# First four attention jobs with unpadded loads and a reordered opening, in a fused linear-attention and two-MLP kernel

## The reference

```python
f = 1.0 / (1.0 + np.exp(-f_logit))
for t in range(S):
    state = f[:, :, t, :, None] * state + np.einsum('bhd,bhe->bhde', k[:, :, t], v[:, :, t])
    y[:, :, t] = np.einsum('bhd,bhde->bhe', q[:, :, t], state)
x = tokens(y)    # (3072, 384)
r = np.maximum(x @ w_in, 0.0);  x = (r * r) @ w_out            # first MLP
h = x @ w_in2;  out = (h * np.tanh(softplus(h))) @ w_out2      # second MLP
```

## Time and profile before

| | |
|---|---|
| median of three runs | 887.02 us |
| the profiled execution's own time | 886.69 us |
| its span, first to last instruction | 885.0 us |
| around the span (886.69 - 885.0) | 1.69 us |
| TensorE matmul busy | 874.3 us, 99% |
| VectorE, ScalarE busy | 597.2 and 594.8 us, 67% each |
| granted TensorE clock | 1.00 |

### The profile page before, as it was taken

The page is one execution under the profiler, slowest core; times in us unless marked ns, Lnnn a source line. Parts: engine busy times, 40 slices in busy tenths (PEclk is TensorE's granted clock), DMA queues, the critical chain, the costliest instruction groups (busy, mean ns, idle before and its releaser), DMA issues.

```text
span 885.0 us, 16260 instructions
## 1 busy us (share of the span) xinstructions
PE 874.3 (99%) x6282; PEld 725.3 (82%) x6282; DVE 597.2 (67%) x1054; ACT 594.8 (67%) x1026; POOL 62.0 (7%) x71
## 2 busy tenths in 40 slices
PE   8899999999999999999999999999999999999998
PEld 7788888888888888888788888888888888888886
DVE  6879545445544444342244799999898898898886
ACT  6776655564546555544566787888887887877874
POOL 0222111111111111110000000000000000000000
PEclk9999999999999999999999999999999999999999
DMA  9644221122212111100233201001001001000100
GB/s 255 203 148 128 76 81 44 44 81 65 66 45 80 44 44 57 46 13 1 92 96 100 90 19 37 37 0 37 37 1 37 36 1 37 36 0 1 36 1 36
DMA packets 25090, 50.64 MB, mean 57 GB/s; under 512 B 2674, under 2 KB 3442, under 8 KB 25010
## 3 DMA queue, kind: packets, MB, share of 16 engines
q1 hardware_dynamic: 25010, 49.56, 18.0%
HBM read 40.11 MB, written 9.44 MB: 56 GB/s over the span
## 4 chain that ended last, share of the span: by engine, by line
PE 98%; DMA 1%; issue 0%; SPq 0%; ACT 0%; DVE 0%; ACTq 0%
PE ps L1069 45%; PE ps L1086 44%; PE ps L1043 2%; PE ps L1013 2%; PE ps L1039 2%; PE ps L991 1%; PE ps L1059 1%; DMA work<-fkq 1%; SPq L284 0%; PE ps L988 0%; PE ps L997 0%; SPq L297 0%; ACT work L497 0%; ACT work L538 0%; SPq L306 0%
## 5 line engine op out<-in xcount | busy, mean ns | idle before, releaser
L1069 PE MATMUL ps<-xs,w_hi 128*128 128x512 f32 x1152 | 359.3, 393 | 1.0 <-issue 1.0
L1069 PEld LDWEIGHTS ps<-xs,w_hi 128*128 128x128 f32 x1152 | 213.0, 188 | 45.0 <-issue 1.6
L1086 PE MATMUL ps<-g_hi,w_lo 128*128 128x512 f32 x576 | 224.1, 389 | 0.0
L1069 PE MATMUL ps<-xs,w_lo 128*128 128x512 f32 x576 | 224.1, 389 | 0.0
L1086 PE MATMUL ps<-g_hi,w_hi 128*128 128x512 f32 x576 | 224.1, 389 | 0.0
L1086 PE MATMUL ps<-g_lo,w_hi 128*128 128x512 f32 x576 | 224.1, 389 | 0.0
L829 DVE TENSOR_TENSOR g_lo<-gb,g_hi 128x512 fp32r<-128x512 f32 x96 | 68.1, 709 | 215.6 <-ACT gb L564 215.6
L559 ACT ACTIVATE rb<-ps 128x512 f32<-128x512 f32 x96 | 57.3, 597 | 161.0 <-PE ps L1069 161.0
L1069 PEld LDWEIGHTS ps<-xs,w_lo 128*128 128x128 f32 x576 | 108.1, 188 | 22.6
L1086 PEld LDWEIGHTS ps<-g_hi,w_hi 128*128 128x128 f32 x576 | 108.1, 188 | 22.5
L1086 PEld LDWEIGHTS ps<-g_hi,w_lo 128*128 128x128 f32 x576 | 108.1, 188 | 22.4
(11 more groups left out here) (82 smaller groups left out, 750.6 us busy)
## 6 DMA issues: line engine op xcount, KB each, us to landing
work<-fkq SPq DMA_DIRECT2D x68, 224.0 KB, 3.7
stage<-w SPq DMA_DIRECT2D x24, 384.0 KB, 3.1
work<-v_tok SPq DMA_DIRECT2D x22, 256.0 KB, 3.9
x_scratch<-yo SPq DMA_DIRECT2D x6, 768.0 KB, 3.8
xs<-x_scratch SPq DMA_DIRECT2D x6, 768.0 KB, 4.4
out<-work SPq DMA_DIRECT2D x17, 256.0 KB, 2.1
yo<-w SPq DMA_DIRECT2D x8, 384.0 KB, 4.6
work<-f_tok SPq DMA_DIRECT2D x4, 224.0 KB, 3.5
```

The costliest lines, as they stand in the source:

```text
L1069: ins = nc.tensor.matmul(bank, w[:, f, k * P:(k + 1) * P], xs[:, half, part, k, :], start=k == 0 and i == 0, stop=k == KT - 1 and i == 2)
L1086: ins = nc.tensor.matmul(ps[:, 5 + d, :], w[:, f, cols], g[:, slot, :], start=f == 0 and i == 0, stop=f == NF - 1 and i == 2)
```

## The change

- Decays of the first four jobs are loaded without padding (128 x 384), and `sums` makes two matmuls for a pair of heads in place of one: 64 columns for rows 0 to 63, 48 for rows 64 to 111, in different column parts of the array.
- Keys and queries of the first four jobs come from a new input `kq_first`, as two loads of 48 partitions each. VectorE first zeroes the gap of the key and query tiles (partitions 32 to 63, 1024 and 1536 elements each), and SP waits for that (`gap_zeroed`).
- Values of all jobs have 112 columns for a pair (48 of the even head, 16 shared zeros, 48 of the odd head) in place of 128.
- SP's order becomes f0 f1 k0 f2 q0 k1 f3 q1 v0 q2 k2 v1 k3 q3 w0 v2 v3; then it waits until v2 has landed before w1, and until v3 has landed before w2.
- VectorE zeroes `am` and `st` after `first_cap(1)` and not at the start, and `first_cap(2)` moves behind `first_queries(0)`.
- ScalarE copies keys(2) and keys(3) out right after their transposes, into `eb`; the wait for increments that this copy had moves to `inverse_decay`.
- TensorE runs `increments(1)` right behind `increments(0)`, ahead of `values(2)`.

```diff
...
+    DP = D + DV
...
-    VALUES = [(0, D), (DV - D, DV)]
+    VALUES = [(0, D), (DV, DP)]
...
-        vb, o = place(o, 2, H, DV)
+        vb, o = place(o, 2, NP, DP)
...
         def f_rows(j):
-            return (fb if j < 2 else eb)[:, j % 2, :, :].rearrange("p n t -> p (n t)")[:, 0:NP * R]
+            return (fb if j < 2 else eb)[:, j % 2, :, :].rearrange("p n t -> p (n t)")[:, 0:DM]
+        def loads(j, places):
+            before = range(j % places, j + 1, places)
+            return 16 * len(before) + 16 * len([i for i in before if i < B])
         def key_rows(j):
+            if j in (2, 3):
+                return eb[:, j % 2, :, :].rearrange("p n t -> p (n t)")[:, 0:NP * R].rearrange("p (n r) -> p n r", r=R)
...
         def v_rows(j):
-            return gb[:, j - 2, :].rearrange("p (h c) -> p h c", c=DV) if j in (2, 3) else vb[:, j % 2, :, :]
+            return gb[:, j - 2, 0:NP * DP].rearrange("p (n c) -> p n c", c=DP) if j in (2, 3) else vb[:, j % 2, :, :]
...
             def load_k(j):
                 if j < NJ:
...
-                    sp.dma_start(kb[0:R, j % 2, :, :].rearrange("p n t -> p (n t)"),
-                                 fkq[j][:, 1, :]).then_inc(k_in[j % 2], 16)
+                    if j < B:
+                        sp.wait_ge(s_["gap_zeroed"], 1)
+                        for e, (lo, hi) in enumerate(PAR):
+                            sp.dma_start(kb[lo:hi, j % 2, :, :].rearrange("p n t -> p (n t)"), kq_first[j, 0, e]).then_inc(k_in[j % 2], 16)
+                    else:
+                        sp.dma_start(kb[0:R, j % 2, :, :].rearrange("p n t -> p (n t)"),
+                                     fkq[j][:, 1, :]).then_inc(k_in[j % 2], 16)
             def load_q(j):
                 if j < NJ:
...
-                    sp.dma_start(qb[0:R, j % 3, :, :].rearrange("p n t -> p (n t)"),
-                                 fkq[j][:, 2, :]).then_inc(q_in[j % 3], 16)
+                    if j < B:
+                        sp.wait_ge(s_["gap_zeroed"], 2)
+                        for e, (lo, hi) in enumerate(PAR):
+                            sp.dma_start(qb[lo:hi, j % 3, :, :].rearrange("p n t -> p (n t)"), kq_first[j, 1, e]).then_inc(q_in[j % 3], 16)
+                    else:
+                        sp.dma_start(qb[0:R, j % 3, :, :].rearrange("p n t -> p (n t)"),
+                                     fkq[j][:, 2, :]).then_inc(q_in[j % 3], 16)
             def load_v(j):
                 if j < NJ:
...
-                    sp.dma_start(v_rows(j).rearrange("p h c -> p (h c)"), v_tok[j % B][t:t + C, :]).then_inc(v_in[j if j < B else j % 2], 16)
+                    sp.dma_start(v_rows(j).rearrange("p n c -> p (n c)"), v_tok[j % B][t:t + C, :]).then_inc(v_in[j if j < B else j % 2], 16)
...
             load_f_tok(0)
             load_f_tok(1)
+            load_k(0)
             load_f_tok(2)
-            load_k(0)
             load_q(0)
+            load_k(1)
             load_f_tok(3)
-            load_k(1)
             load_q(1)
+            load_v(0)
             load_q(2)
-            load_v(0)
             load_k(2)
             load_v(1)
             load_k(3)
...
             load_w(0)
             load_v(2)
             load_v(3)
+            sp.wait_ge(v_in[2], 16)
             load_w(1)
             load_f(4)
+            sp.wait_ge(v_in[3], 16)
             load_w(2)
             load_k(4)
             load_q(4)
...
+                if j < B + 2:
+                    act.wait_ge(s_["kv_done"], j - 1)
...
-                elif j >= 2:
-                    act.wait_ge(s_["kv_done"], j - 1)
...
             def x1_hi(j):
...
             first_decay(3)
...
             x1_hi(0)
+            keys_out(2)
             weights_hi(0)
             x1_hi(1)
+            keys_out(3)
             ends_out(2)
             ends_out(3)
             x1_hi(2)
             x1_hi(3)
             weights_hi(1)
-            keys_out(2)
-            keys_out(3)
             weights_hi(2)
...
         def _(dve):
+            nc.vector.memset(kb[Q:GAP, :, :, :], 0.0).then_inc(s_["gap_zeroed"], 1)
+            nc.vector.memset(qb[Q:GAP, :, :, :], 0.0).then_inc(s_["gap_zeroed"], 1)
...
-            dve.wait_ge(s_["set_up"], 2)
-            parts = halves(am[:, :, :, :, :].rearrange("p j b n t -> p (j b n) t"))
-            nc.vector.memset(parts[0:HC, :, 2, :], 0.0).then_inc(s_["st_zeroed"], 1)
-            nc.vector.memset(parts[HC:P, :, 0, :], 0.0).then_inc(s_["st_zeroed"], 1)
-            nc.vector.memset(st[:], 0.0).then_inc(s_["st_zeroed"], 1)
+            def no_scores():
+                parts = halves(am[:, :, :, :, :].rearrange("p j b n t -> p (j b n) t"))
+                nc.vector.memset(parts[0:HC, :, 2, :], 0.0).then_inc(s_["st_zeroed"], 1)
+                nc.vector.memset(parts[HC:P, :, 0, :], 0.0).then_inc(s_["st_zeroed"], 1)
+            def no_states(b):
+                nc.vector.memset(st[:, b:b + 2, :, :], 0.0).then_inc(s_["st_zeroed"], 1)
             def first_cap(j):
...
             def first_keys(j):
-                dve.wait_ge(k_in[j % 2], 16 * (j // 2 + 1))
+                dve.wait_ge(k_in[j % 2], loads(j, 2))
...
             def first_queries(j):
-                dve.wait_ge(q_in[j % 3], 16 * (j // 3 + 1))
+                dve.wait_ge(q_in[j % 3], loads(j, 3))
...
             def mask(j):
...
-                    dve.wait_ge(s_["st_zeroed"], 3)
+                    dve.wait_ge(s_["st_zeroed"], 2)
...
             def queries(j):
...
-                dve.wait_ge(q_in[j % 3], 16 * (j // 3 + 1))
+                dve.wait_ge(q_in[j % 3], loads(j, 3))
...
-                    dve.wait_ge(s_["st_zeroed"], 3)
+                    dve.wait_ge(s_["st_zeroed"], 4)
...
             first_cap(0)
             first_cap(1)
-            first_cap(2)
+            no_scores()
+            no_states(0)
             first_keys(0)
             first_queries(0)
+            first_cap(2)
+            no_states(2)
             first_keys(1)
             first_queries(1)
             first_cap(3)
...
             def sums(j):
...
                 for n in range(NP):
-                    ins = nc.tensor.matmul(ps_sums(j)[:, n, :], f_rows(j)[:, R * n:R * n + R], tri, start=True, stop=True)
+                    for (lo, hi), at in zip(ROWS, (0, D)):
+                        ins = nc.tensor.matmul(ps_sums(j)[lo:hi, n, :], f_rows(j)[:, 2 * D * n + at:2 * D * n + at + hi - lo], tri,
+                                               start=True, stop=True, skip_group_check=True, tile_position=(0, lo))
                 ins.then_inc(s_["sums_done"], 1)
...
-            RESULT = [(h // 4, h % 4, h, Q * (h % 2)) for h in range(H)]
-            RESULT += [(2, h // 2, h, Q - Q * (h % 2)) for h in list(range(0, H, 2)) + list(range(1, H, 2))]
+            RESULT = [(h // 4, h % 4, h, (DP - Q) * (h % 2)) for h in range(H)]
+            RESULT += [(2, h // 2, h, Q + (D - Q) * (h % 2)) for h in list(range(0, H, 2)) + list(range(1, H, 2))]
...
-                        ins = nc.tensor.matmul(ps_kv(j)[lo:hi, n, :], key_rows(j)[:, n, lo:hi], v_rows(j)[:, 2 * n + i // 2, v0:v1],
+                        ins = nc.tensor.matmul(ps_kv(j)[lo:hi, n, :], key_rows(j)[:, n, lo:hi], v_rows(j)[:, n, v0:v1],
...
             keys(3)
             scores(3)
             increments(0)
+            increments(1)
             values(2)
             values(3)
-            increments(1)
             increments(2)
             increments(3)
...
+    def first(a):
+        return a[:, :, 0:P].reshape(b, h // 2, 2, P, d).transpose(0, 2, 4, 1, 3).reshape(b, 2, d, h // 2 * P)
...
-        "f_tok": lay(jobs(f_logit, 30.0)[0:b].reshape(b, GAP + d, h // 2, P).transpose(0, 3, 2, 1)).reshape(b, P, -1),
+        "f_tok": lay(f_logit[:, :, 0:P].transpose(0, 2, 1, 3)).reshape(b, P, h * d),
+        "kq_first": lay(np.stack([first(k), first(q)], axis=1)),
...
```

More of the change, by code:

```diff
@@ L14, with attention_ffn @@
 GAP = 64
-def attention_ffn(nc, fkq, f_tok, v_tok, vT, w1, w2, out):
+def attention_ffn(nc, fkq, f_tok, kq_first, v_tok, vT, w1, w2, out):
     B, H, D, S = vT.shape
@@ L187, in ps_h2 @@
             return ps[:, t % 5, :]
-        names = """set_up zeroed st_zeroed const_ready causal_ready
+        names = """set_up gap_zeroed zeroed st_zeroed const_ready causal_ready
             ft_exped ft_capped ft_logged sums_done m_ready
@@ L468, in decayed_keys @@
             def decayed_keys(j):
-                pool.wait_ge(k_in[j % 2], 16 * (j // 2 + 1))
+                pool.wait_ge(k_in[j % 2], loads(j, 2))
                 pool.wait_ge(s_["scanned"], j - B + 1)
@@ L1042, in values @@
                 for d, i, h, at in RESULT:
-                    ins = nc.tensor.matmul(y[Q * i:Q * i + Q, d, :], v[:, h, at:at + Q], am[:, j % 2, h % 2, h // 2, :],
+                    ins = nc.tensor.matmul(y[Q * i:Q * i + Q, d, :], v[:, h // 2, at:at + Q], am[:, j % 2, h % 2, h // 2, :],
```

(14 more changed lines are left out.)

## The result

The changed kernel takes 889.81 us (median of 6, 888.68 to 891.12) against 886.92 us (median of 6, 885.14 to 887.30) for the kernel before: ratio 1.0039, 95% interval 1.0028 to 1.0049. That is 2.9 us slower, where 0.75 us faster was forecast; the time lies above the range. The profiled execution took 889.12 us, span 887.4 us, 2.4 us longer than the span before.

A forecast was written before the change was run, and what follows sets the result against it. TensorE was taken as the bound, its opening paced by program loading. Terms summed to 0 to -1.9 us, likeliest -0.75: 885.9 us for the profiled execution, 886.3 against 887.02 for the median; range 884.6 to 888.6.

The forecast's parts named there:

- The front: Opening up to scores(1): the DMA wait is replaced by the cap's later place, 0.45 us later; bounds -0.2 to +0.9.
- the cap's new place: VectorE, opening: first_cap(2) behind first_queries(0) delays growth(1) from 8.86 to 9.9 us, making scores(1) 0.45 us later.
- only keys(1) waits for a load: VectorE, opening: only keys(1) waits for a load, 0.77 us ahead of 10.08, and that wait goes.
- Halves of `sums`: TensorE, opening: two half matmuls overlap, +0.05 us for each `sums`; if not, +2 us for each of the first two.
- The pace of program loading: TensorE, second half of opening: 16 KB instruction pieces set the pace; third usable at 27.4, up1(0) at 27.9, -0.75 us.
- the forecast break at increments(0): TensorE, opening: 0.5 to 1.5 us gap inside or right behind increments(0), second program piece usable between 21.0 and 23.5.
- Behind them TensorE is full and its work is the same, so the time follows one for one.: From up1(0) and down1(0) on: any shift of their starts passes unchanged into the kernel's time.
- The jump: Jump halfway, 1.05 us idle TensorE before; target 64 instructions later in its piece; priced 0, with 0 to +1 us.
- a changed gap behind the jump: Sign listed as showing the forecast wrong: TensorE's gap behind the halfway jump differs from before; no size given.
- VectorE behind it: Ahead of down1(0): VectorE's g1_lo(0) caps the gain between 0.7 and 2.5 us, but does not bind at -0.75.
- The rivals: Opening: loading doesn't bind, 884.8 us (0.22); nothing comes of it, 887.2 (0.16); piece stuck behind loads, 890.6 (0.12).
- Rival 3: Opening: a program piece stuck behind loads w1 to k4, up1(0) at 32.2, +3.6 us, 890.6 us; chance 0.12.

## Why the prediction was wrong

- *The front.* Right in sum: scores(1) at 14.19 (14.15). VectorE's keys(1) were at 10.84, released by ScalarE, and the load that held them before was no longer late. That the cap's new place costs was borne out by the run that undid it: about 0.9 us. The text's "only keys(1) waits for a load" was a misreading; the kernel before's VectorE also waits 0.15 us for queries(1) and 0.33 for keys(2).
- *Halves of `sums`.* Right: 1.09 us for the 16 records of sums(2), where 8 whole ones took 1.04; the halves overlap. The first two `sums` can't show it (3.15 against 3.63 us in the first pair of profiles): over all fourteen they took 2.00 to 3.51 us with halves and 2.21 to 3.63 with whole ones.
- *The pace of program loading.* Right in place and sign: break inside increments(2), packet at 24.7 (24.8), resumption at 27.43 (27.4). The second piece came at the early end of its bounds, so the forecast break at increments(0) didn't come. The closeness of the third's time is luck in part: w1 was issued at 18.09, 1 us later than worked out, the loads kept the DMA engines full to about 26.2 and not to 24.8, so the packet did not wait for all of them, and the same program had it 0.8 us earlier in another execution.
- *"Behind them TensorE is full and its work is the same, so the time follows one for one."* **This step failed.** The work was the same, its rate wasn't. I priced the 2.8 us gap by its length alone; the price was the half clock behind it, 1.64 us in the profiled execution. By the mean clocks most others had twice the half-clock time; what that cost is not shown. No rival had it. The Trainium skill ("TensorE: Matmul & The Clock Gate", "HAM oscillation — how this bites in real kernels") says that a wait for data between bursts of matmuls puts the clock back, so that the next burst starts cold. The trace agrees, and adds that gaps of 1.94, 1.81 and even 1.33 us can do it, and that one of 2.94 us and one of 2.28 us did not.
- *The jump.* **This term was mis-sized:** priced 0 with 0 to +1, it measured +1.29 in the profiled execution (0.49 and 0.80). The mechanism of the 0.80, a short remainder of a piece, stood in the text, and a changed gap behind the jump was among the signs of being wrong; I took the end of its bounds that left it out.
- *VectorE behind it.* Right that it doesn't bind; it bound, by 0.25 and 0.27 us, in two of the runs with a short gap.
- *The rivals.* Rival 3 had the sign, but by another mechanism: no piece was stuck. Its price of 3.6 us was close by chance.

Open: why the clock falls in one execution and not in another of the same program. Only profiled executions show where it fell; the others have a mean alone, so for them it is shown that there was half clock and argued that it lay behind the same gap. What makes the gap at the jump longer, and what decides whether the piece behind it comes in time, was not measured.

## What to carry to other kernels

An idle stretch of TensorE of some 1.9 us or more in front of dense matmuls cost its length and, in most executions, 1.6 us of slow restart behind it: price both, and of two places for a gap choose the one behind which TensorE waits anyway. Look for gaps of "issue" inside a group of instructions that waits for nothing, count the instructions between two of them, and if it is a constant, treat program loading as a transfer of its own, which comes sooner when fewer loads are issued ahead of it. A load that is put off to make room must still land before its own user: a hold with the weight tile last left the kernel 0.15% above the kernel before, an earlier one with the weight tile first 0.21% below it.

## What the runs showed of the hardware that was not expected

- Gaps of 1.8 to 4.2 us on TensorE were followed by 3.4 us of granted clock 0.50 in 7 of 9 cases, whatever the cause of the gap: missing program (3.23, 2.76, 2.54 and 1.94 us), ScalarE (4.22, 2.94 and 1.81 us). It stayed full behind the other 2.94 us and behind the 2.28 us ahead of scores(4). Of the shorter gaps, one of 1.33 us was followed by it; those at the jump, 1.04 to 1.60 us, never in 14 profiles. The clock fell between 0.5 us before TensorE resumed and 1.0 us after.
- A packet of 16 KB of instructions comes later when more loads are issued ahead of it: 1216 KB of them moved one from 18.5 to 20.4 us, and 832 KB fewer moved another from 24.7 to 22.3 us, where the same program varied by 0.8 us. It does not wait for all of them: behind the packet at 24.7 the DMA engines stayed full of loads for 1.3 us.
- In all five profiles with two breaks in the opening, 126 matmuls lay between them, one piece with their weight loads and waits (in the one without SP's waits the trace names VectorE for the first). 64 instructions more ahead of the jump brought a second gap behind it, hundreds of microseconds later, in a kernel that had none.
